# Scaling k and q of a couple's first pair one step earlier, ahead of the second pair's decay

## What is computed

```python
# attention with a decaying state, for each batch and head
for t in range(S):
    state = alpha[:, :, t, :, None] * state + np.einsum('bhd,bhe->bhde', k[:, :, t], v[:, :, t])
    y[:, :, t] = np.einsum('bhd,bhde->bhe', q[:, :, t], state)
x = y as (3072 tokens, 384)
# first feed-forward layer
x = (np.maximum(x @ moe_w_in, 0.0) ** 2) @ moe_w_out          # 384 -> 2048 -> 384
# second feed-forward layer
h = x @ moe2_w_in
x = (h * (1.0 / (1.0 + np.exp(-h)))) @ moe2_w_out             # 384 -> 2048 -> 384
```

## Time and profile before

| | us |
|---|---|
| median of 3 runs | 886.68 |
| lowest and highest run | 886.6, 889.64 |
| the profiled execution's own time | 888.62 |
| its span, first to last instruction | 887.0 |
| PE busy in the span | 862.5 (97%) |
| DVE, ACT, POOL busy | 544.8, 436.5, 106.1 |
| mean granted clock of TensorE | 0.99 |

### The profile page before, as it was taken

How to read it: one execution, slowest core, us unless ns; L and a number is a source line. 1 busy time by engine, 2 the same in 40 slices (tenths; PEclk the granted TensorE clock), 3 DMA queues, 4 the chain that set the end, 5 groups by cost and what they waited for, 6 DMA issues and landing times.

```text
span 887.0 us, 17687 instructions
## 1 busy us (share of the span) xinstructions
PE 862.5 (97%) x6834; PEld 714.2 (81%) x6834; DVE 544.8 (61%) x1090; ACT 436.5 (49%) x788; POOL 106.1 (12%) x127
## 2 busy tenths in 40 slices
PE   7999999998999899989999999999999999999998
PEld 6778788887778777878888888888888888888898
DVE  7789888877576657653234565555855446766620
ACT  5756654454445445534567654445543336545510
POOL 3463200000000000000165003002020003000000
PEclk9999999999999899989999999999999999999999
DMA  8884444334242414100321353000130000110010
GB/s 169 232 235 110 107 114 113 79 84 106 55 107 71 97 31 101 55 18 11 116 72 54 66 113 89 1 1 1 37 107 0 1 1 1 36 37 1 1 48 28
DMA packets 134204, 60.04 MB, mean 68 GB/s; under 512 B 81824, under 2 KB 129312, under 8 KB 134112
## 3 DMA queue, kind: packets, MB, share of 16 engines
q1 hardware_dynamic: 130800, 58.14, 26.6%
q10 hardware_dynamic: 3312, 0.69, 0.4%
HBM read 45.02 MB, written 9.44 MB: 61 GB/s over the span
## 4 chain that ended last, share of the span: by engine, by line
PE 83%; DVE 8%; issue 4%; ACT 3%; SPq 1%; DMA 1%; DVEq 0%; ACTq 0%
PE h_ps L1239 20%; PE z_ps L1210 17%; PE h_ps L1196 17%; PE z_ps L1275 11%; PE jobs L1275 7%; PE jobs L1295 3%; DVE decay L1784 3%; DVE decay L1769 2%; DVE kp L1738 2%; PE jobs L1062 1%; PE jobs L1073 1%; PE h_ps L1295 1%; ACT g L1507 1%; ACT g L1513 1%; DVE kp L1802 1%
## 5 line engine op out<-in xcount | busy, mean ns | idle before, releaser
L1507 ACT ACTIVATE g<-h_ps 128x512 f32<-128x512 f32 x96 | 57.1, 595 | 170.0 <-PE h_ps L1196 167.9
L1899 DVE TENSOR_TENSOR g_lo<-g,g_hi 128x512 fp32r<-128x512 f32 x96 | 68.1, 712 | 101.9 <-ACT g L1513 101.8
L1601 ACT ACTIVATE sum<-sum 128x512 f32<-128x512 f32 x96 | 60.6, 631 | 137.2 <-DVE sum L1960 112.2
L1960 DVE TENSOR_TENSOR sum<-h_ps,sum 128x512 f32<-128x512 f32 x120 | 82.9, 691 | 56.5 <-PE h_ps L1239 53.9
L1196 PE MATMUL h_ps<-x_hi,win_hi 128*128 128x512 f32 x288 | 114.1, 396 | 2.5 <-DVE x_lo L1891 0.9
L1210 PE MATMUL z_ps<-g_hi,wout_hi 128*128 128x512 f32 x282 | 115.4, 409 | 0.0
L1196 PE MATMUL h_ps<-x_lo,win_hi 128*128 128x512 f32 x288 | 112.3, 390 | 0.0
L1196 PE MATMUL h_ps<-x_hi,win_lo 128*128 128x512 f32 x288 | 112.2, 390 | 0.0
L1210 PE MATMUL z_ps<-g_hi,wout_lo 128*128 128x512 f32 x282 | 112.2, 398 | 0.0
L1210 PE MATMUL z_ps<-g_lo,wout_hi 128*128 128x512 f32 x282 | 111.9, 397 | 0.0
L1239 PE MATMUL h_ps<-s_hi,t_hi 128*128 128x512 f32 x264 | 103.1, 390 | 0.2 <-DVE sum L1960 0.2
(11 more groups left out here) (185 smaller groups left out, 1597.4 us busy)
## 6 DMA issues: line engine op xcount, KB each, us to landing
z_scratch<-z_sb SPq DMA_DIRECT2D x18, 256.0 KB, 2.7
pre<-z_scratch SPq DMA_DIRECT2D x18, 256.0 KB, 3.8
v_sb<-in_v SPq DMA_DIRECT2D x44, 96.0 KB, 2.5
out_x<-z_stage SPq DMA_DIRECT2D x80, 48.0 KB, 1.7
nat_a<-in_alpha SPq DMA_DIRECT2D x40, 88.0 KB, 2.3
nat_k<-in_k SPq DMA_DIRECT2D x40, 88.0 KB, 2.2
nat_q<-in_q SPq DMA_DIRECT2D x40, 88.0 KB, 2.3
nat_a<-in_alpha SPq DMA_DIRECT2D x40, 80.0 KB, 2.2
```

Source lines behind the costliest of these rows:

```text
L1507: nc.scalar.activation(g[f % 2][:], h_ps[f % 2][:], ACT.Relu).then_inc(act_made, 1)
L1601: nc.scalar.activation(at[:], at[:], ACT.Silu).then_inc(silu_made, 1)
L1899: nc.vector.tensor_tensor(low, g[f % 2][:], high.bitcast(F32), ALU.subtract).then_inc(g_lo_made, 1)
L1960: nc.vector.tensor_tensor(to[:], h_ps[(PRODUCTS * n + r) % 2][:], other[:], ALU.add).then_inc(summed, 1)
```

## The change

For couples from pair 14 on, stage KQ of the first pair is put at base - 2 in place of base - 1. Nothing else is edited.

```diff
     base = 4 * first - 20
     outputs = 4 if base % NF == 12 else 5
     if n % 2 == 0:
-        return base + {"A": -4, "KQ": -1, "S": 0, "I": 3, "Y": outputs}[kind]
+        return base + {"A": -4, "KQ": -2, "S": 0, "I": 3, "Y": outputs}[kind]
     return base + {"A": -2, "KQ": 1, "S": 3, "I": outputs, "Y": 7 if n == LASTP else 8}[kind]
```

## The result

| | us |
|---|---|
| changed kernel, median of 4 runs | 875.06 (874.11 to 877.34) |
| kernel before, median of 4 runs beside it | 888.02 (886.6 to 889.64) |
| ratio, 95% interval | 0.9857 [0.9827, 0.9887] |
| profiled execution of the changed kernel, its span | 874.47, 872.8 |

The kernel is 1.4% faster. Run once more on another chip it took 876.0 (6 runs) against 889.99, ratio 0.9826 [0.9791, 0.9860].

A forecast was written before the change was run, and what follows sets the result against it. PE, busy 97%, was held by waits for q at the scores (12.0 us) and the low clock after them. Five couples' gains, 13.61 us including 6.7 of clock, taken from 888.62 gave 875.0; range 870.0 to 881.0.

The forecast's parts named there:

- PE waits for q at the scores: At L1062 PE waits for VectorE's scaling of q, 12.0 us in 5 waits, all of which go.
- The idle time takes k and q; the shift is 1.09 and 1.27 us: On VectorE 3.48 us of work fills idle time ahead of low_g(base - 2), which starts only 1.09 or 1.27 us later.
- low_g being later costs nothing: Its taker, second_product(base - 2), stands behind the scores on PE; without that cover it would cost up to 1.27 us.
- The addition of Y comes next: Before step base + 1 PE newly waits for VectorE's addition of pair n - 1's output, 5.1 us in all.
- The gains by couple: Earlier starts of step base + 1: 1.46, 2.64, 4.10, 1.28 and 4.13 us for couples 14 to 22, sum 13.61.
- The clock: PE's low clock behind the scores of n = 16, 18, 22 goes, worth 6.7 us; new waits bring none.
- The Trainium skill's rule: Low clock's penalty is half the throttled time: 3.05 us against 2.66 at n = 18, sum about 1 us larger.
- The load of k and q: SyncE's loads move one step up and cost nothing, with 28 us of slack for q of pair 16.
- No new wait: Rival: the addition of Y isn't late, the 5.1 us of new waits go too, 869.9 us; chance 0.08.
- No effect: Rival: the scores wait for something else of the same time, 886 to 889 us; chance 0.06.
- late loads: Rival: k or q arrive late and hold up VectorE; at 4 us each 895 us, slower; chance 0.03.

The follow-up runs named there:

- filled wait: Kernel before, with PE doing eight unread matmuls of 512 columns while it waits for q, k and q in their old place: 882.75 us, ratio 0.9921.
- k and q behind low_g: Changed kernel, but in step base - 2 VectorE does low_g first, then k and q, then the second pair's decay: 894.05 us, ratio 1.0054.
- late bound: Changed kernel, with ScalarE taking the bound of each second pair's decay one step later, behind the copies of Y: 869.53 us, repeated 868.26.
- loads alone: Kernel before, with only SyncE's loads of k and q a step earlier and VectorE's order kept: 889.3 us, ratio 0.9992.
- two couples alone: Kernel before, with k and q moved for couples 14 and 20 only: 884.25 us, ratio 0.9927.

## Why the prediction was right

It was 875.0, the median is 875.06, the profiled execution 874.47. The mechanism held term by term, as the list shows. That the numbers agree to 0.1 us is luck: the four runs lie 3.2 us apart, and between steps 36 and 95 the gain was 293.12 - 279.12 = 14.0 us, 0.4 more than the sum.

- *PE waits for q at the scores.* Shown: the wait went with the move, and the filled wait names the scaling of q as its end.
- *The idle time takes k and q; the shift is 1.09 and 1.27 us.* At couple 18 Y's last matmul ends 4.35 us earlier than before (289.09 against 293.44), and its second copy starts at 292.46 in place of 295.73, so it has moved by 292.46 - (295.73 - 4.35) = 1.08 us. At couple 16 the same reckoning gives 1.22. The run with k and q behind low_g shows what it costs without this idle time.
- *low_g being later costs nothing.* No wait of PE at L1210 stands in its list.
- *The addition of Y comes next.* Five new waits: 1.33, 0.57, 1.34, 0.57 and 1.03 us against 1.38, 0.67, 1.40, 0.67 and 1.01. The sum is 4.84 for 5.1. Most of the difference is the 0.10 us that I took for PE's start: VectorE's last addition ends at 293.62 and PE starts at 293.68, 0.06 later. The late bound shows that it comes over ScalarE.
- *The gains by couple.* From the starts of step base + 1, each against the couple's own beginning: 1.51, 2.74, 4.15, 1.37, 4.17, in all 13.94 for 13.61.
- *The clock.* 1.00 at all five places, as taken. The filled wait puts its price at 7.15 us, for 6.7 (1.37, 2.66 and 2.65). Up to the start of step base + 2 the filled wait saved 1.48, 2.83 and 2.87 us at these couples, in all 7.2: my three terms end at the first matmul of step base + 1, and the low clock lasted on behind it (at n = 18 from 295.80 to 302.63, the matmul is at 302.18). This was the least certain term, and the runs show why: what happens behind a wait is not fixed by its length (below). In the trace read, none of the new waits brought it. One run of four took 877.34 us with a mean clock of 0.998; it has no trace, so where its clock fell stays open.
- *The Trainium skill's rule* ("TensorE: Matmul & The Clock Gate", "HAM oscillation — how this bites in real kernels": the penalty is half the throttled time) gives an upper figure. In the run with k and q behind low_g the clock was at half for 3.4 us four times (0.79 in 8 us), by the rule 6.8 us, and 6.1 were measured. In the kernel before the low clock lasted 3.41 + 6.83 + 6.83 = 17.07 us, longer than the 6.10 I read at n = 18; by the rule that is 8.5 us, and 7.15 were measured. Part of such a stretch PE was idle in any case (0.48 us at n = 18), and not all of its work took twice as long: the 32 scores took 1.13 us for 0.69, 1.6 times.
- *The load of k and q.* The run with the loads alone: no effect either way.
- *The rivals.* "No new wait" would have been 869.9. The late bound makes it so. It gives 6.3 to 6.4 us and not the 5.1 of the waits, for the 0.3 us more a wait that this figure left out, and 869.53 (with its late start) and 868.26 were measured. "No effect" and "late loads" had nothing behind them.

The 1.9 us between median and profiled execution before, which I put down to the clock, are not shown to be that: the run of 886.68 has no trace. With one run more the median before was 888.02, next to the 888.62 of the profile, and most of the gap was gone.

## What to carry to other kernels

Work can be moved ahead at a small cost into the place where its engine is idle (here 1.1 or 1.2 us of shift for 3.5 us of work), and a place one instruction further along may cost more than the move brings: look for the bracket with the idle time, not only for the wait to be removed. Ask what was hidden behind the wait that goes, and follow it over every in-order queue; here a bookkeeping activation that nobody waited for soon held up two copies behind it, and taking it out of the way gave another 6.3 us. Count a wait of PE as longer than the profile's idle time says, here by 0.3 us. When two profiled executions are compared, look first whether they start and end alike: 1.4 us at the start and up to 2.3 at the end came and went here whatever the kernel. Where PE's waits bring the lower clock, count its loss as a term of its own: it was half of the gain.

## What the runs showed of the hardware

The same wait of PE may or may not be followed by 1.2 GHz. A wait of 1.94 us was (n = 16 before), 1.92 in the same place wasn't (two couples alone). One of 2.84 wasn't at n = 14 in the kernel before, and one of the same length there was in the run with the loads alone. One of 3.39 wasn't in the run with k and q behind low_g, while 2.83 and 3.74 there were. None of the waits of the couples up to 1.4 us was, in any trace read. The clock can fall while PE still waits (0.48 us before the scores of n = 18, 0.40 before those of n = 22) or behind the wait (1.64 us after the start of the scores of n = 16).

The clock explains most of the spread of the kernel before. Its fastest run of the 27 (884.48) has a mean clock of 0.996, its slowest (896.48) 0.983. An estimate of what each lost, one minus the clock times the span, gives 3.5 and 15.2 us, 11.7 of the 12.0 between them; with this loss taken off, the 27 runs lie 3.5 us apart. The changed kernel's runs lie 3.2 us (4 runs) and 2.3 us (6 runs) apart.
